# Attention and token/channel mixer on one core: w_ch1 fetched and split earlier, x split in the last two pairs, token products between the last turns

## The chip, the cores and the metric

The kernel runs on one core of one Trainium2 chip. The metric is device time in microseconds (us), the median of the timed executions. Engines are called PE (matmul), ACT, DVE, POOL (GpSimd) and SP (here only a DMA queue).

## The reference

Attention comes first, for 4 batches of 8 heads with 576 rows of 64 columns, all float32:

```python
q_rot, k_rot = (rotate(q), rotate(k))
scores = scale * np.matmul(q_rot, k_rot.transpose(0, 1, 3, 2))
scores = scores - np.max(scores, axis=-1, keepdims=True)
attn = np.exp(scores)
attn = attn / (np.sum(attn, axis=-1, keepdims=True) + 1e-09)
x = np.matmul(attn, v)            # heads side by side: 4 x 576 x 512
```

Then a mixer, with w_tok1 576x256, w_tok2 256x576, w_ch1 512x1536, w_ch2 1536x512:

```python
xt = x.transpose(0, 2, 1)
h = np.maximum(xt @ w_tok1, 0.0) @ w_tok2
u = x + h.transpose(0, 2, 1)
h2 = np.maximum(u @ w_ch1, 0.0) @ w_ch2
return u + h2
```

## The kernel before

**Two stages.** `attention` works through 16 pairs of heads (p = 0 to 15). `mixer` then works through 4 batches. Each engine has its own instruction list, written out by hand; there is no planner. Engines meet only at semaphores.

**One pair.** A pair has nine score tiles, i = 0 to 8. For each, PE makes the scores (`score`, L589 and L593), DVE takes the row maximum (`maximum`, L801), ACT the exponent (`exponent`, L715), PE turns the result (`turn`, ten transposes, L531), ACT and DVE copy the two halves out of PSUM (`copy_up` L724, `copy_low` L810), and PE multiplies by v (`values`, twenty matmuls, L633). There is one pair of banks for turned tiles: `turn` of a tile waits until both copies of the tile before are done. Tiles 7 and 8 are turned within the next pair's scores. The turned q of pair p+1 passes through `copy_q` (ACT, L705) and a DMA `moved_q` issued by SP (`move`, L422), and the first score of pair p+1 waits for that DMA. SP also waits in its list for `copy_v` (POOL, L500), to load v of pair p+1, ahead of these moves.

**Exact products out of rounded parts.** A float32 product of the mixer is made of three passes: operands are split into a rounded part ("hi", an ACT copy to float32r, `split_hi`) and the rest ("lo", a subtraction, `split_lo`, on DVE or POOL). `ChannelWeights` holds w_ch1: eight half chunks come by DMA (L156), `split_hi` (L162) rounds each half, `split_lo` (L169) subtracts a whole chunk of 128x1536. `TokenProducts` holds batch 0's x: five tiles t = 0 to 4, `split_hi` L204, `split_lo` L209 (L213 for the last, half one), and `products` (L221 to L224, six matmuls of 512 columns a tile, four for the last).

**The handover.** After the pair loop PE does: turn 7, values 5 and 6, products of x tiles 0 and 1, turn 8, values 7 and 8, products of x tiles 2 to 4. Then the mixer: `h_hi` (ACT, L1307) and `h_lo` (DVE, `token_lo`, L1494) read these sums; `u_unit` 0 to 3 (five transposes L1141, then twelve matmuls L1148); `hidden(0)` (L1116 to L1118), whose chunk c waits for `u_lo` of chunk c (DVE, L1500) and for `split_lo` of w_ch1's chunk c. SP loads w_ch2 in the meantime and POOL forms sums of it (L1091).

**Where the w_ch1 work lies.** The loads are issued in pairs 4 to 11. ACT rounds chunks 0 and 1 in pairs 13 and 14, chunks 2 and 3 after the loop. POOL subtracts chunks 0 and 1 at the end of pairs 14 and 15. DVE subtracts chunk 2 at the end of attention and chunk 3 within the mixer, between `u_lo` 1 and `u_lo` 2. The place of chunks 2 and 3 of w_ch1's rounded part is shared with `prob_a`, the exponents of tiles 0 to 4.

**Where the x work lies.** ACT rounds tiles 0 and 1 in pair 15 (tile 0 after `copy_up` of tile 8, tile 1 at its end, ahead of `copy_up` 6), the others after the loop. POOL subtracts tiles 0 and 1, DVE tiles 2 to 4.

Of the kernel before, what the change touches and what calls it, by code (L numbers as in the profile page):

```python
# [17 lines left out]
P = 128  # L18
# [43 lines left out]
def build(nc, q, k, v, w_tok1, w_tok2, w_ch1, w_ch2, rope, x_scratch, out):  # L62
    with ExitStack() as whole:
# [13 lines left out]
        w_ch1_lo = sb(whole, "w_ch1_lo", [P, CT, CH], F32R)  # L77
        with ExitStack() as placed:
            sb(placed, "w_ch1_first", [P, CT // 2, CH])
            prob_a = sb(placed, "prob_a", [P, CT // 2 * CH])  # L80
        wc1 = [sb(whole, "w_ch1_hi", [P, CT, CH], F32R), w_ch1_lo]
# [27 lines left out]
        with ExitStack() as ctx:  # L109
            first = attention(nc, ctx, whole, sb, slot, rest, ident, stage_or_x, raw_qk, rope_sb, rope_half, prob_a, token, wt1,  # L110
                              wt2, w1, x_stored, q, k, v, w_tok1, w_tok2, w_ch1, rope, x_scratch)
# [29 lines left out]

Attention = namedtuple("Attention", "sync gpsimd tensor scalar vector last_store buffers_left values_left slot_left")
Mixer = namedtuple("Mixer", "sync gpsimd tensor scalar vector first_token_hi")
# [83 lines left out]

def attention(nc, ctx, whole, sb, slot, rest, ident, stage_or_x, raw_qk, rope_sb, rope_half, prob_a, token, wt1, wt2, w1, x_stored,
              q, k, v, w_tok1, w_tok2, w_ch1, rope, x_scratch):
# [25 lines left out]
    MOVED_COLS = {"q": (slice(0, W), slice(0, W)), "k": (slice(HALF, S), slice(0, HALF))}  # L255
    sb(ctx, "spare_too", [P, 4576])

# [143 lines left out]
    def sync(sp):  # L401
# [45 lines left out]
        for p in range(N):  # L447
            if not no(p + 1):
                sp.wait_ge(v_copied, 2 * p + 2)
                load("v", p + 1)  # L450
            if not no(p + 1):
                sp.wait_ge(scores, p * TILES + G + 1)
            move("k", 0, p + 1)
            move("q", 0, p + 1)
            store(p - 1)
            load_next("k", p + 3)
            sp.wait_ge(scores, (p + 1) * TILES)
            move("k", 1, p + 1)
            move("q", 1, p + 1)
            load_next("q", p + 3)  # L460
            if 1 <= p <= len(chunks):
                for dst, part in chunks[p - 1][0]:
                    sp.dma_start(dst, part).then_inc(w_in[p - 1], 16)
            if 4 <= p < 4 + 2 * CT:
                w1.load(sp, w_ch1, (p - 4) // 2, p % 2)
            if p == 10:

                sp.wait_ge(x_stored, STORED * HP)
                sp.wait_ge(w_lo_done, len(PIECES))
                token.load_x(sp, 0, range(0, 2), ())  # L470
            if p == 11:
                token.load_x(sp, 0, range(2, HP), ())
            if p == 12:
                token.load_x(sp, 0, ())

    def gpsimd(pool):
# [35 lines left out]
        for p in range(N):  # L512
            copy_v(p, "B")
            if not no(p + 2):
                rotate(pool, "k", p + 2)
            copy_v(p + 1, "A")
            if not no(p + 2):
                rotate(pool, "q", p + 2)
            if p == N - 1:
                token.split_lo(pool, 0, 0)  # L520
                token.split_lo(pool, 0, 1)
            if 3 <= p < 3 + len(PIECES):
                weights_lo(p - 3)
            if N - 2 <= p < N:
                w1.split_lo(pool, p - (N - 2))

    def tensor(pe):
# [143 lines left out]

        first, p = slot[0], N
        turn(p - 1, 7)
        values(p - 1, 5)
        values(p - 1, 6)
        pe.wait_ge(exped, N * TILES - 1)
        token.products(pe, 0, 0, first).then_inc(token.x_used, 1)
        token.products(pe, 0, 1, first).then_inc(token.x_used, 1)
        turn(p - 1, 8)
        values(p - 1, 7)  # L680
        values(p - 1, 8)
        token.products(pe, 0, 2, first).then_inc(token.x_used, 1)
        token.products(pe, 0, 3, first).then_inc(token.x_used, 1)
        token.products(pe, 0, 4, first).then_inc(token.sums_ready, 1)

    def slot_left(pe, k):
# [9 lines left out]
    def scalar(act, h1_of_batch_0):  # L696
# [43 lines left out]
        for p in range(N):  # L740
            exponent(p, 0)
            exponent(p, 1)
            copy_up(p - 1, 8)
            if N - 3 <= p < N - 1:
                w1.split_hi(act, p - (N - 3), 0)
            if p == N - 1:
                act.wait_ge(products, 4 * N)
                token.split_hi(act, 0, 0)
            exponent(p, 2)
            copy_up(p, 0)  # L750
            exponent(p, 3)
            copy_up(p, 1)
            copy_up(p, 2)
            exponent(p, 4)
            copy_up(p, 3)
            exponent(p, 5)
            exponent(p, 6)
            copy_q(p + 1)
            copy_up(p, 4)
            exponent(p, 7)  # L760
            copy_up(p, 5)
            exponent(p, 8)
            if 3 <= p < 3 + len(PIECES):
                weights_hi(p - 3)
            if N - 3 <= p < N - 1:
                w1.split_hi(act, p - (N - 3), 1)
            if p == N - 1:
                token.split_hi(act, 0, 1)
            copy_up(p, 6)
            copy_up(p, 7)  # L770

        p = N
        token.split_hi(act, 0, 2)
        copy_up(p - 1, 8)
        token.split_hi(act, 0, 3)
        token.split_hi(act, 0, 4)
        w1.split_hi(act, 2, 0)
        w1.split_hi(act, 2, 1)
        w1.split_hi(act, 3, 0)
        act.wait_ge(token.sums_ready, 1)  # L780
        h1_of_batch_0(act)
        w1.split_hi(act, 3, 1)

    def vector(dve):
# [26 lines left out]

        def guard(p, h):
            if no(p):
                return
            t0, t1 = HEADS[h]
            dve.wait_ge(o_added, p * TILES + t1)
            dve.tensor_tensor(guarded[p % 2][:, t0:t1], output(h)[:, :, D], eps[:, t0:t1], ALU.add).then_inc(guard_done, 1)

        def invert(p, h):
            if no(p):  # L820
                return
            t0, t1 = HEADS[h]
            dve.wait_ge(guard_done, 2 * p + "AB".index(h) + 1)
            dve.reciprocal(inverse[p % 2][:, t0:t1], guarded[p % 2][:, t0:t1]).then_inc(inv_done, 1)

        def normalise(p, h):
            if no(p):
                return
            a, (t0, t1) = "AB".index(h), HEADS[h]
            dve.wait_ge(inv_done, 2 * p + a + 1)  # L830
            if p > 0:
                dve.wait_ge(x_stored, p * STORED)
            dve.tensor_tensor(x_pair[:, 1 - a:NG, a, :], output(h)[:, :, 0:D],
                              inverse[p % 2][:, t0:t1].unsqueeze(2).broadcast_to([P, t1 - t0, D]), ALU.mult).then_inc(x_done, 1)

        dve.memset(raw["q"][0:TAIL, 1, G, :], 0.0).then_inc(zero_halves, 1)
# [11 lines left out]
        for p in range(N):  # L848
            maximum(p, 0)
            copy_low(p - 1, 7)  # L850
            maximum(p, 1)
            normalise(p - 1, "A")
            copy_low(p - 1, 8)
            maximum(p, 2)
            maximum(p, 3)
            copy_low(p, 0)
            guard(p - 1, "B")
            copy_low(p, 1)
# [5 lines left out]
            copy_low(p, 3)  # L864
            invert(p - 1, "B")
            normalise(p - 1, "B")
            copy_low(p, 4)
            maximum(p, 7)
            maximum(p, 8)
            copy_low(p, 5)  # L870
            guard(p, "A")
            copy_low(p, 6)
            invert(p, "A")

        p = N
        copy_low(p - 1, 7)
        normalise(p - 1, "A")
        copy_low(p - 1, 8)
        token.split_lo(dve, 0, 2)
        token.split_lo(dve, 0, 3)  # L880
        guard(p - 1, "B")
        invert(p - 1, "B")
        token.split_lo(dve, 0, 4)
        normalise(p - 1, "B")
        w1.split_lo(dve, 2)

# [9 lines left out]
    def buffers_left(sp):  # L896

        sp.wait_ge(scores, N * TILES)

    def values_left(pool):  # L900

        pool.wait_ge(o_added, N * TILES)

    return Attention(sync=sync, gpsimd=gpsimd, tensor=tensor, scalar=scalar, vector=vector,
                     last_store=last_store, buffers_left=buffers_left, values_left=values_left, slot_left=slot_left)


def mixer(nc, ctx, sb, slot, ident, h, h1, pieces, token, wt2, wc1, w1, w1_sums, w1_parts, h_early, x_stored, first, w_ch1, w_ch2,
# [580 lines left out]
    def vector(dve):  # L1489
# [126 lines left out]

        token_lo(0, slot[0])

        def body(b, begins=False, last=False):
            if begins:  # L1620
                for c in range(CT):
                    u_lo(b, c)
                    if c == 1:
                        w1.split_lo(dve, 3)
                for n in range(len(WEIGHTS)):
                    w2_lo(n)
                los(b, 0, 3)
                add_u(b, 0)
            else:
                shares(b)  # L1630
# [132 lines left out]
```

## Time and profile before

| what | us |
|---|---|
| median of 3 runs | 621.48 (621.3 to 623.23) |
| profiled execution, its own time | 619.15 |
| its span (first to last instruction) | 617.2 |
| PE busy | 595.7 (97%) |
| DVE busy | 443.9 (72%) |
| ACT busy | 387.3 (63%) |
| POOL busy | 274.6 (44%) |

The profiled execution was 2.33 us shorter than the median, and 1.95 us of it lie outside the span. The granted clock was 0.998 of full speed. Attention ends and the mixer begins at about 275 us of the span. PE's busy time includes matmuls that overlap, so 97% tells only that its gaps are few.

### The profile page before, as it was taken

The page shows a single profiled execution, that of the slowest core. Times are in us where ns is not written, and L with a number is a line of the kernel's source. Part 1 is how long each engine was busy: PE and PEld are TensorE (multiplying, and loading weights), DVE is VectorE, ACT ScalarE, POOL GpSimd, SP SyncE. Part 2 cuts the span into 40 slices and gives each one's busy share as a digit, 9 for nine tenths or more (in the row PEclk, how much of TensorE's full clock was granted, in tenths as well). Part 3 has the DMA queues.
Part 4 walks back from the last instruction along what each step waited for, and adds up shares of the span by engine and source line. Part 5 has one row for each costly group of instructions (what it writes and reads, how often), then busy time and mean ns, then how long its engine had stood idle before and what let it go on. Part 6 is the DMA issues. An engine that isn't in the chain of part 4 may idle for free.

```text
span 617.2 us, 19511 instructions
## 1 busy us (share of the span) xinstructions
PE 595.7 (97%) x7796; PEld 543.1 (88%) x7796; DVE 443.9 (72%) x844; ACT 387.3 (63%) x725; POOL 274.6 (44%) x240
## 2 busy tenths in 40 slices
PE   2999999999999999989999999999999999999997
PEld 1788788788888888879999999999999999999996
DVE  5588788778888888855568876389735699364895
ACT  2566677776666677753736556775567766567753
POOL 4666677776666663348000016820038600168100
PEclk9999999999999999999999999999999999999999
DMA  4235445455456642270005320000310003200002
GB/s 136 74 95 152 127 110 135 133 136 137 135 137 171 169 127 72 58 235 1 1 1 205 86 77 1 1 2 6 107 51 0 0 0 85 78 0 1 1 2 78
DMA packets 49870, 48.18 MB, mean 78 GB/s; under 512 B 12800, under 2 KB 42048, under 8 KB 49792
## 3 DMA queue, kind: packets, MB, share of 16 engines
q1 hardware_dynamic: 49488, 47.00, 26.8%
q8 instruction: 58, 0.95, 0.6%
q14 instruction: 20, 0.16, 0.1%
q10 hardware_dynamic: 304, 0.07, 0.1%
HBM read 30.24 MB, written 9.44 MB: 64 GB/s over the span
## 4 chain that ended last, share of the span: by engine, by line
PE 93%; DVE 2%; DMA 1%; ACT 1%; issue 0%; DVEq 0%
PE rest L633 15%; PE slot L593 12%; PE rest L531 9%; PE slot L1116 8%; PE slot L1118 8%; PE slot L1117 8%; PE rest L1116 6%; PE rest L1118 6%; PE rest L1117 6%; PE slot L1148 2%; PE slot L531 2%; PE slot L589 2%; PE rest L1148 2%; DMA moved_q<-turned_q 1%; PE rest L224 1%; PE rest L221 1%
## 5 line engine op out<-in xcount | busy, mean ns | idle before, releaser
L801 DVE TENSOR_REDUCE neg_max<-slot 128x1 f32<-128x576 f32 x144 | 106.4, 755 | 21.6 <-PE slot L593 16.8
L1107 POOL TENSOR_TENSOR w_ch_part<-w_ch_sums,w_ch_part 128x512 fp32r<-128x512 f32 x21 | 31.0, 1476 | 180.3 <-ACT w_ch_part L1358 180.3
L1422 ACT ACTIVATE pieces<-h 128x288 fp32r<-128x288 f32 x168 | 73.8, 444 | 49.8 <-PE slot L1118 24.5
L633 PE MATMUL rest<-v,pt 128*64 128x65 f32 x2880 | 102.4, 225 | 0.0
L633 PEld LDWEIGHTS rest<-v,pt 128*64 128x64 f32 x2880 | 91.2, 138 | 10.6 <-ACT pt L724 6.2
L810 DVE COPY pt<-rest 128x320 f32<-128x320 f32 x144 | 70.1, 487 | 33.7 <-PE rest L531 33.2
L724 ACT ACTIVATE pt<-rest 128x320 f32<-128x320 f32 x144 | 62.7, 435 | 49.2 <-PE rest L531 48.2
L593 PE MATMUL slot<-turned_k,turned_q 64*128 64x288 f32 x256 | 86.3, 442 | 4.4 <-DMA moved_q<-turned_q 2.0
L593 PE MATMUL slot<-moved_k,moved_q 64*128 64x288 f32 x256 | 86.6, 443 | 0.0
L1513 DVE TENSOR_TENSOR pieces<-h,pieces 128x288 fp32r<-128x288 f32 x168 | 74.4, 453 | 9.3 <-ACT pieces L1422 8.8
L715 ACT ACTIVATE prob_a<-slot,neg_max 128x576 f32<-128x576 f32 x80 | 59.3, 741 | 17.5 <-DVE neg_max L801 14.4
L715 ACT ACTIVATE prob_b<-slot,neg_max 128x576 f32<-128x576 f32 x64 | 47.5, 742 | 12.9 <-DVE neg_max L801 10.3
L593 PEld LDWEIGHTS slot<-turned_k,turned_q 64*128 64x128 f32 x256 | 41.1, 192 | 10.0 <-ACT prob_a L715 4.4
L500 POOL COPY v<-raw_v 128x320 f32<-128x320 f32 x32 | 14.5, 452 | 78.4 <-PE rest L633 78.4
L531 PEld LDWEIGHTS rest<-ident,prob_a 64*128 64x128 f32 x800 | 35.0, 142 | 14.6 <-ACT pt L724 7.5
L593 PEld LDWEIGHTS slot<-moved_k,moved_q 64*128 64x128 f32 x256 | 41.1, 192 | 7.2 <-ACT turned_q L705 6.0
L1580 DVE TENSOR_TENSOR h<-h 128x288 f32<-128x288 f32 x96 | 42.6, 452 | 3.9 <-ACT h L1321 3.8
L361 POOL TENSOR_TENSOR by_sin<-raw_qk,rope_sb 128x640 f32<-128x640 f32 x29 | 44.9, 1550 | 0.0
L360 POOL TENSOR_TENSOR by_cos<-raw_qk,rope_sb 128x640 f32<-128x640 f32 x29 | 44.8, 1544 | 0.0
L531 PE MATMUL rest<-ident,prob_a 64*128 64x64 f32 x800 | 40.5, 230 | 0.8 <-ACT pt L724 0.8
L1358 ACT ACTIVATE w_ch_part<-w_ch_sums 128x512 fp32r<-128x512 f32 x42 | 26.5, 630 | 13.9 <-PE slot L1118 11.6
L531 PEld LDWEIGHTS rest<-ident,prob_b 64*128 64x128 f32 x640 | 28.1, 139 | 7.8 <-ACT pt L724 1.8
(236 smaller groups left out, 1761.3 us busy)
## 6 DMA issues: line engine op xcount, KB each, us to landing
moved_q<-turned_q SPq DMA_DIRECT2D x31, 160.0 KB, 2.7
raw_qk<-in_q_dram SPq DMA_DIRECT2D x16, 256.0 KB, 2.7
raw_v<-in_v_dram SPq DMA_DIRECT2D x16, 256.0 KB, 2.9
x_scratch<-x_pair SPq DMA_DIRECT2D x16, 256.0 KB, 2.7
stage_or_x<-x_scratch SPq DMA_DIRECT2D x16, 256.0 KB, 4.1
raw_qk<-in_k_dram SPq DMA_DIRECT2D x15, 256.0 KB, 2.9
w_ch_whole<-in_moe_w_ch_dram SPq DMA_DIRECT2D x8, 384.0 KB, 3.5
w_ch_A_whole<-in_moe_w_ch_dram SPq DMA_DIRECT2D x4, 768.0 KB, 7.8
```

The source lines that it names most:

```text
L531: return pe.matmul(to, x, ident[rows, rows], start=True, stop=True, is_transpose=True, skip_group_check=True)
L593: mm = pe.matmul(s[:, r, 0:HALF], x[:, cols], w, start=True, stop=True, skip_group_check=True)
L633: mm = pe.matmul(to[cols], pt_of(p, i)[:, j, cols], w, start=(j == 0), stop=(j == G), skip_group_check=True)
L715: act.activation(prob[i].rearrange("p (f n) -> p f n", f=2), score_slot(p, i)[:, :, 0:HALF], ACT.Exp, bias=neg_max[p % 2][:, i:i + 1]).the ...
L724: act.activation(pt_of(p, i)[:, :, top], rest[:, 0, 0:NG * D].rearrange("p (j n) -> p j n", j=NG), ACT.Copy).then_inc(up_done, 1)
L801: dve.tensor_reduce(neg_max[p % 2][:, i:i + 1], score_slot(p, i)[:, :, 0:HALF], AX.XY, ALU.max, negate=True).then_inc(maxed, 1)
L810: dve.tensor_copy(pt_of(p, i)[:, :, low], rest[:, 1, 0:NG * D].rearrange("p (j n) -> p j n", j=NG)).then_inc(low_done, 1)
L1116: pe.matmul(ps, lhs[0], rhs[0], start=first, stop=False, skip_group_check=True)
L1117: pe.matmul(ps, lhs[0], rhs[1], start=False, stop=False, skip_group_check=True)
L1118: return pe.matmul(ps, lhs[1], rhs[0], start=False, stop=last, skip_group_check=True)
L1422: act.activation(pieces[:, ring(m), 0, :], source[WEIGHTS[n]][:, ft, :], ACT.Copy).then_inc(piece_hi, 1)
L1513: dve.tensor_tensor(pieces[:, ring(m), 1, :], source[WEIGHTS[n]][:, ft, :], f32(pieces[:, ring(m), 0, :]), ALU.subtract).then_inc(piece_lo, 1)
```

## The change

1. `prob_a` gets a place of its own, so that w_ch1's chunks 2 and 3 can be rounded while attention runs. The load of w_ch2 waits also for turn 4 of the last pair.
2. The loads of w_ch1 are issued in pairs 3 to 10.
3. ACT rounds one chunk of w_ch1 in each of pairs 12 to 15: the first half after `copy_up` 8 of the pair before, the second at the end of the pair (in pair 15 behind `copy_up` 7).
4. POOL subtracts all four chunks, at the ends of pairs 13, 14 and 15 and after the loop. DVE subtracts none.
5. ACT rounds x tile 0 in pair 14 before exponent 5 and tile 1 at pair 14's end; tile 2 in pair 15 before exponent 5, tile 3 before `copy_up` 4, tile 4 after the loop. POOL subtracts tiles 0 to 3 (two in each of pairs 14 and 15), DVE tile 4. In pair 15 `copy_up` 6 is ahead of exponent 8.
6. PE, after the loop: products of tile 0, turn 7, values 5 and 6, products of tile 1, turn 8, products of tiles 2 to 4, values 7 and 8.
7. DVE's guard, reciprocal and normalisation of the last head run after the mixer's `token_lo`.

The diff, cut to its core:

```diff
-        with ExitStack() as placed:
-            sb(placed, "w_ch1_first", [P, CT // 2, CH])
-            prob_a = sb(placed, "prob_a", [P, CT // 2 * CH])
...
-    sb(ctx, "spare_too", [P, 4576])
+    sb(ctx, "spare_too", [P, 4576 - NG * S])
+    prob_a = sb(ctx, "prob_a", [P, NG * S])
...
-            if 4 <= p < 4 + 2 * CT:
-                w1.load(sp, w_ch1, (p - 4) // 2, p % 2)
+            if 3 <= p < 3 + 2 * CT:
+                w1.load(sp, w_ch1, *divmod(p - 3, 2))
...
-            if p == N - 1:
-                token.split_lo(pool, 0, 0)
-                token.split_lo(pool, 0, 1)
+            if p >= N - 2:
+                for t in range(2):
+                    token.split_lo(pool, 0, 2 * (p - (N - 2)) + t)
...
-            if N - 2 <= p < N:
-                w1.split_lo(pool, p - (N - 2))
+            if p > N - CT:
+                w1.split_lo(pool, p - (N - CT) - 1)
+        w1.split_lo(pool, CT - 1)
...
         first, p = slot[0], N
+        pe.wait_ge(exped, N * TILES - 1)
+        token.products(pe, 0, 0, first).then_inc(token.x_used, 1)
         turn(p - 1, 7)
         values(p - 1, 5)
         values(p - 1, 6)
-        pe.wait_ge(exped, N * TILES - 1)
-        token.products(pe, 0, 0, first).then_inc(token.x_used, 1)
         token.products(pe, 0, 1, first).then_inc(token.x_used, 1)
         turn(p - 1, 8)
-        values(p - 1, 7)
-        values(p - 1, 8)
         token.products(pe, 0, 2, first).then_inc(token.x_used, 1)
         token.products(pe, 0, 3, first).then_inc(token.x_used, 1)
         token.products(pe, 0, 4, first).then_inc(token.sums_ready, 1)
+        values(p - 1, 7)
+        values(p - 1, 8)
...
-            if N - 3 <= p < N - 1:
-                w1.split_hi(act, p - (N - 3), 0)
-            if p == N - 1:
-                act.wait_ge(products, 4 * N)
-                token.split_hi(act, 0, 0)
+            if p >= N - CT:
+                w1.split_hi(act, p - (N - CT), 0)
...
             copy_up(p, 3)
+            if p == N - 2:
+                act.wait_ge(products, 4 * N)
+                token.split_hi(act, 0, 0)
+            if p == N - 1:
+                token.split_hi(act, 0, 2)
             exponent(p, 5)
             exponent(p, 6)
             copy_q(p + 1)
+            if p == N - 1:
+                token.split_hi(act, 0, 3)
             copy_up(p, 4)
             exponent(p, 7)
             copy_up(p, 5)
+            if p == N - 1:
+                copy_up(p, 6)
             exponent(p, 8)
             if 3 <= p < 3 + len(PIECES):
                 weights_hi(p - 3)
-            if N - 3 <= p < N - 1:
-                w1.split_hi(act, p - (N - 3), 1)
+            if N - CT <= p < N - 1:
+                w1.split_hi(act, p - (N - CT), 1)
+            if p == N - 2:
+                token.split_hi(act, 0, 1)
+            if p < N - 1:
+                copy_up(p, 6)
+            copy_up(p, 7)
             if p == N - 1:
-                token.split_hi(act, 0, 1)
-            copy_up(p, 6)
-            copy_up(p, 7)
+                w1.split_hi(act, CT - 1, 1)
 
         p = N
-        token.split_hi(act, 0, 2)
+        token.split_hi(act, 0, 4)
         copy_up(p - 1, 8)
-        token.split_hi(act, 0, 3)
-        token.split_hi(act, 0, 4)
-        w1.split_hi(act, 2, 0)
-        w1.split_hi(act, 2, 1)
-        w1.split_hi(act, 3, 0)
         act.wait_ge(token.sums_ready, 1)
         h1_of_batch_0(act)
-        w1.split_hi(act, 3, 1)
...
         normalise(dve, p - 1, "A")
+        dve.wait_ge(token.x_lo_done, G)
+        token.split_lo(dve, 0, G)
         copy_low(p - 1, 8)
-        token.split_lo(dve, 0, 2)
-        token.split_lo(dve, 0, 3)
-        guard(p - 1, "B")
-        invert(p - 1, "B")
-        token.split_lo(dve, 0, 4)
-        normalise(p - 1, "B")
-        w1.split_lo(dve, 2)
+
+    def last_output(dve):
+        for step in (guard, invert, normalise):
+            step(dve, N - 1, "B")
...
         sp.wait_ge(scores, N * TILES)
+        sp.wait_ge(turned, (N - 1) * TILES + G + 1)
...
         token_lo(0, slot[0])
+        first.last_output(dve)
...
-                    if c == 1:
-                        w1.split_lo(dve, 3)
```

## Rows read from the trace of the kernel before

**Rows 1.** The page: the chain that ended last, by engine
```profile
PE 93%; DVE 2%; DMA 1%; ACT 1%; issue 0%; DVEq 0%
```

**Rows 2.** Waits of PE, whole span: who for whom, us in total, times, longest
```profile
PE slot L593 <- DMA moved_q<-turned_q: 2.0, 2, 1.3
PE rest L531 <- ACT pt L724: 1.6, 2, 0.9
...
PE slot L1116 <- DVE ut_lo L1500: 1.0, 1, 1.0
PE slot L1148 <- DVE h_lo L1494: 0.9, 1, 0.9
```

**Rows 3.** Timeline of PE, 246 to 296: start, us, engine, line, operation, tiles, [idle before]
```profile
263.63 0.53 PE L531 MATMUL rest<-ident,prob_b 64*128 64x64 f32 x10
265.02 0.53 PE L531 MATMUL rest<-ident,prob_b 64*128 64x64 f32 x10 [0.86 <-ACT pt L724]
265.47 1.39 PE L633 MATMUL rest<-v,pt 128*64 128x65 f32 x40
266.79 0.50 PE L221 MATMUL slot<-x_parts,w_tok_hi 128*128 128x512 f32 x1
267.13 0.40 PE L223 MATMUL slot<-x_parts,w_tok_hi 128*128 128x512 f32 x1
...
269.78 0.53 PE L531 MATMUL rest<-ident,prob_b 64*128 64x64 f32 x10
...
275.51 0.71 PE L1141 MATMUL slot<-ident,stage_or_x 128*128 128x128 f32 x5
277.09 0.39 PE L1148 MATMUL slot<-w_tok_hi,h_hi 128*128 128x256 f32 x1 [0.87 <-DVE h_lo L1494]
...
278.78 0.71 PE L1141 MATMUL slot<-ident,stage_or_x 128*128 128x128 f32 x5
279.24 0.36 PE L1148 MATMUL slot<-w_tok_hi,h_hi 128*128 128x256 f32 x1
...
286.51 0.30 PE L1117 MATMUL slot<-ut_lo,w_ch_hi 128*128 128x288 f32 x1
286.65 0.29 PE L1118 MATMUL slot<-ut_hi,w_ch_lo 128*128 128x288 f32 x1
287.92 0.40 PE L1116 MATMUL slot<-ut_hi,w_ch_hi 128*128 128x288 f32 x1 [0.98 <-DVE ut_lo L1500]
```

**Rows 4.** Timeline of DVE, 216 to 300
```profile
282.60 4.53 DVE L169 TENSOR_TENSOR w_ch_lo<-w_ch_whole,w_ch_hi 128x1536 fp32r<-128x1536 f32 x1
```

**Rows 5.** Timeline of POOL, 216 to 300
```profile
240.06 0.45 POOL L500 COPY v<-raw_v 128x320 f32<-128x320 f32 x1 [1.10 <-PE rest L633]
...
281.99 3.54 POOL L1091 TENSOR_TENSOR w_ch_S_whole<-w_ch_S_whole,w_ch_A_whole 128x1536 f32<-128x1536 f32 x1
```

**Rows 6.** Timeline of ACT, 216 to 300
```profile
245.86 0.70 ACT L705 ACTIVATE turned_q<-slot 128x640 f32<-128x640 f32 x1 [0.23 <-PE slot L531]
...
249.83 0.45 ACT L724 ACTIVATE pt<-rest 128x320 f32<-128x320 f32 x1
...
261.08 0.44 ACT L724 ACTIVATE pt<-rest 128x320 f32<-128x320 f32 x1 [0.29 <-PE rest L531]
...
264.00 0.64 ACT L204 ACTIVATE x_parts<-stage_or_x 128x512 fp32r<-128x512 f32 x1
264.52 0.45 ACT L724 ACTIVATE pt<-rest 128x320 f32<-128x320 f32 x1
```

**Rows 7.** Timeline of PE, 244 to 252: turn 7 of pair 14
```profile
250.41 0.50 PE L531 MATMUL rest<-ident,prob_b 64*128 64x64 f32 x10
```

**Rows 8.** POOL's subtractions of w_ch1 chunks: ns min/median/max, first and last start
```profile
L169 POOL TENSOR_TENSOR w_ch_lo<-w_ch_whole,w_ch_hi x2: 3458/3470/3482, 249.6 to 265.9; 128x1536 fp32r<-128x1536 f32 x2
```

**Rows 9.** The 62 moves of turned q and k (L422)
```profile
DMA to landing us min/median/max: 1.9/2.7/4.8
```

**Rows 10.** Timeline of SP's queue, 40 to 80
```profile
60.03 2.53 SPq L432 DMA_DIRECT2D x_scratch<-x_pair  x2
```

More of the change, by code:

```diff
@@ L109, in build @@
         with ExitStack() as ctx:
-            first = attention(nc, ctx, whole, sb, slot, rest, ident, stage_or_x, raw_qk, rope_sb, rope_half, prob_a, token, wt1,
+            first = attention(nc, ctx, whole, sb, slot, rest, ident, stage_or_x, raw_qk, rope_sb, rope_half, token, wt1,
                               wt2, w1, x_stored, q, k, v, w_tok1, w_tok2, w_ch1, rope, x_scratch)
@@ L139, in _ @@
                     then.vector(dve)
-Attention = namedtuple("Attention", "sync gpsimd tensor scalar vector last_store buffers_left values_left slot_left")
+Attention = namedtuple("Attention", "sync gpsimd tensor scalar vector last_output last_store buffers_left values_left slot_left")
 Mixer = namedtuple("Mixer", "sync gpsimd tensor scalar vector first_token_hi")
@@ L225, in products, with attention @@
         return mm
-def attention(nc, ctx, whole, sb, slot, rest, ident, stage_or_x, raw_qk, rope_sb, rope_half, prob_a, token, wt1, wt2, w1, x_stored,
+def attention(nc, ctx, whole, sb, slot, rest, ident, stage_or_x, raw_qk, rope_sb, rope_half, token, wt1, wt2, w1, x_stored,
               q, k, v, w_tok1, w_tok2, w_ch1, rope, x_scratch):
@@ L764, in scalar, with guard, invert, normalise @@
                 weights_hi(p - 3)
-            if N - 3 <= p < N - 1:
-                w1.split_hi(act, p - (N - 3), 1)
+            if N - CT <= p < N - 1:
[5 more added lines that the diff above has]
+            copy_up(p, 7)
             if p == N - 1:
-                token.split_hi(act, 0, 1)
-            copy_up(p, 6)
-            copy_up(p, 7)
+                w1.split_hi(act, CT - 1, 1)
         p = N
-        token.split_hi(act, 0, 2)
+        token.split_hi(act, 0, 4)
         copy_up(p - 1, 8)
-        token.split_hi(act, 0, 3)
-        token.split_hi(act, 0, 4)
-        w1.split_hi(act, 2, 0)
-        w1.split_hi(act, 2, 1)
-        w1.split_hi(act, 3, 0)
         act.wait_ge(token.sums_ready, 1)
         h1_of_batch_0(act)
-        w1.split_hi(act, 3, 1)
+    def guard(dve, p, h):
+        if no(p):
+            return
+        t0, t1 = HEADS[h]
+        dve.wait_ge(o_added, p * TILES + t1)
+        dve.tensor_tensor(guarded[p % 2][:, t0:t1], output(h)[:, :, D], eps[:, t0:t1], ALU.add).then_inc(guard_done, 1)
+    def invert(dve, p, h):
+        if no(p):
+            return
+        t0, t1 = HEADS[h]
+        dve.wait_ge(guard_done, 2 * p + "AB".index(h) + 1)
+        dve.reciprocal(inverse[p % 2][:, t0:t1], guarded[p % 2][:, t0:t1]).then_inc(inv_done, 1)
+    def normalise(dve, p, h):
+        if no(p):
+            return
+        a, (t0, t1) = "AB".index(h), HEADS[h]
+        dve.wait_ge(inv_done, 2 * p + a + 1)
+        if p > 0:
+            dve.wait_ge(x_stored, p * STORED)
+        dve.tensor_tensor(x_pair[:, 1 - a:NG, a, :], output(h)[:, :, 0:D],
+                          inverse[p % 2][:, t0:t1].unsqueeze(2).broadcast_to([P, t1 - t0, D]), ALU.mult).then_inc(x_done, 1)
     def vector(dve):
@@ L810, in copy_low @@
             dve.tensor_copy(pt_of(p, i)[:, :, low], rest[:, 1, 0:NG * D].rearrange("p (j n) -> p j n", j=NG)).then_inc(low_done, 1)
[L812 to L834, printed above, removed]
         dve.memset(raw["q"][0:TAIL, 1, G, :], 0.0).then_inc(zero_halves, 1)
@@ L851, in vector @@
             maximum(p, 1)
-            normalise(p - 1, "A")
+            normalise(dve, p - 1, "A")
             copy_low(p - 1, 8)
@@ L856, in vector @@
             copy_low(p, 0)
-            guard(p - 1, "B")
+            guard(dve, p - 1, "B")
             copy_low(p, 1)
@@ L864, in vector @@
             copy_low(p, 3)
-            invert(p - 1, "B")
-            normalise(p - 1, "B")
+            invert(dve, p - 1, "B")
+            normalise(dve, p - 1, "B")
             copy_low(p, 4)
@@ L870, in vector @@
             copy_low(p, 5)
-            guard(p, "A")
+            guard(dve, p, "A")
             copy_low(p, 6)
-            invert(p, "A")
+            invert(dve, p, "A")
         p = N
         copy_low(p - 1, 7)
-        normalise(p - 1, "A")
+        normalise(dve, p - 1, "A")
+        dve.wait_ge(token.x_lo_done, G)
+        token.split_lo(dve, 0, G)
         copy_low(p - 1, 8)
-        token.split_lo(dve, 0, 2)
-        token.split_lo(dve, 0, 3)
-        guard(p - 1, "B")
-        invert(p - 1, "B")
-        token.split_lo(dve, 0, 4)
-        normalise(p - 1, "B")
-        w1.split_lo(dve, 2)
+    def last_output(dve):
+        for step in (guard, invert, normalise):
+            step(dve, N - 1, "B")
     def last_store(sp):
@@ L904, in attention @@
     return Attention(sync=sync, gpsimd=gpsimd, tensor=tensor, scalar=scalar, vector=vector,
-                     last_store=last_store, buffers_left=buffers_left, values_left=values_left, slot_left=slot_left)
+                     last_output=last_output, last_store=last_store, buffers_left=buffers_left, values_left=values_left, slot_left=slot_left)
 def mixer(nc, ctx, sb, slot, ident, h, h1, pieces, token, wt2, wc1, w1, w1_sums, w1_parts, h_early, x_stored, first, w_ch1, w_ch2,
```

## Prediction

> **What bounds the kernel now.** I read the chain of waits first: 93% of it is PE [rows 1], so only PE's gaps and added PE work can move the time. The second view is PE's waits: beside start-up it waits 2.0 us for the `moved_q` DMA (two times), 1.6 for ACT's copies, 1.0 for `ut_lo` and 0.9 for `h_lo` [rows 2]. The third view is PE's timeline about 275 us, where three of these gaps stand in one handover: 0.86, 0.87 and 0.98 us [rows 3]. Everything that the change moves on ACT, DVE and POOL is off the chain, unless it closes one of these or opens a new one. So the sum has at most some 3 us to win out of 619.15 us of the profiled execution (span 617.2 and 1.95 around it). The median was 2.33 above that execution; I carry the difference over unchanged.
>
> **Gap one, before turn 7.** Turn 7 waits for `copy_up` 6, and ACT has exponent 8 and the rounding of x tile 1 ahead of it. Turn 6 starts at 263.63; a turn gives way to the next work after 0.45 (265.02 to 265.47), so PE is free at 264.08 and starts at 265.02 [rows 3]: 0.94 lost. Afterwards products of tile 0 stand there. They need exponent 7, which ACT has finished before 264.00 [rows 6], and x tile 0 split in pair 14. They last longer than the copy that turn 7 then waits for, which now goes ahead of exponent 8. Gain 0.94.
>
> **Gap two, before the first mixer products.** The sums are followed by the five transposes at 275.51. In the next unit the L1148 matmuls follow their transposes after 0.46 (278.78 to 279.24), here after 1.58 (275.51 to 277.09), because ACT's `h_hi` and DVE's `h_lo` come between [rows 3]: 1.12 lost. Afterwards values 7 and 8 follow the sums. They are 40 matmuls of the kind that took 1.32 (265.47 to 266.79), and with 0.46 of transposes this covers 1.78, more than the 1.58 needed [rows 3]. Gain 1.12. With ACT free of w_ch1 and DVE's last-head steps behind `token_lo`, nothing is queued before the two splits. What is late next is x_done for unit 3, about 1 us after `token_lo`, while PE needs it three units (over 6 us) on: hidden.
>
> **Gap three, in the first hidden tile.** Matmuls there follow each other after 0.14 (286.51, 286.65); the next comes at 287.92, so 1.13 is lost [rows 3]. It waits for `ut_lo` of chunk 2, which stands in DVE's list behind the subtraction of w_ch1's chunk 3, 282.60 to 287.13 [rows 4]. That subtraction goes to POOL, before the mixer. Chunk 2 is then ready long before, and chunk 3's splits have 2.4 us of hidden matmuls (18 by 0.13) to finish in. Gain 1.13. Sum of gains 0.94 + 1.12 + 1.13 = 3.19.
>
> **Cost one: one more switch of kind.** Products go in three blocks instead of two. The first product holds PE for 0.34 (266.79 to 267.13), the eleven behind it 0.24 each (267.13 to 269.78) [rows 3]: 0.10 to enter a block. Leaving one has no row of its own; from 0 to the 0.10 of entering, I take 0.1. Cost 0.2.
>
> **Cost two: x tile 1 at the end of pair 14.** The rounding of x tile 1 holds ACT for 0.52 (264.00 to 264.52), and PE's turn begins 0.05 after the copy behind it is over (264.52 + 0.45, against 265.02) [rows 3, 6]. In pair 14 the copy behind it is `copy_up` 6, now at 249.83 for 0.45 [rows 6]. Moved by 0.52 it ends at 250.80, and turn 7 can start at 250.85 instead of 250.41 [rows 7]. That is 0.44 on PE, the only engine without slack. The exponents of pair 15 behind it move along with PE and cost nothing more. The bounds are 0 (PE late for another reason) and the whole 0.52.
>
> **Other ACT insertions.** x tile 0 before exponent 5 of pair 14 uses 0.52, in front of exponents that wait for DVE's maxima anyway; ACT has another 0.23 idle before `copy_q` [rows 6]. I find `copy_q` unmoved. In pair 15, x tiles 2 and 3 move `copy_up` 4 (idle 0.29 before it [rows 6]) by about 0.3, to the very edge of turn 5. Value 0, at worst 0.3. w_ch1's first halves stand where such halves stand now in pairs 13 and 14, and the second halves of pairs 12 to 14 likewise, with no wait of PE among rows 2 that names them: 0. Pair 15's second half is behind `copy_up` 7 and covered by values and products.
>
> **POOL and SP.** The subtraction of chunk 0 (3.47 [rows 8]) now stands in pair 13 ahead of `copy_v` for pair 14, which ran at 240.06 [rows 5]; it comes out near 242.4. SP waits for it in order, then issues v's load and pair 15's `moved_k`, both now near 243 to 245, and only then `moved_q`, which waits for `copy_q` (ends 246.56 [rows 6]) anyway. So the queue isn't late, but v's load is now just ahead of `moved_q`. That DMA lands after 2.7 at the median and 4.8 at worst [rows 9], and at 2.7 it lands just as PE wants it. I take 0, since a stall here would hide the 0.44 of cost two; the upper end is 2.1 - 0.4 = 1.7. POOL's sums of w_ch2 start when their loads land and values 8 is over, about as before. The added wait for turn 4 on SP is over before the last score, for which SP waits already: 0. w_ch1's loads keep their number and size; one lands beside pair 4's start instead of one beside pair 12's: 0 to the 1.3 of the longest such stall [rows 2]. Moving `prob_a` changes no instruction.
>
> **A rule against the change.** DVE's subtraction of 4.53 ran while POOL's L1091 was busy to 285.53 (281.99 + 3.54), and ended 1.60 after that [rows 4, 5]: it had stood still until POOL was done. The Trainium skill, "SBUF — State Buffer", section "Who interferes with whom", has the rule: a DVE operation with two SBUF inputs and a GpSimd operation that reads SBUF exclude each other for a whole instruction, and which starts second waits. These rows agree. After the change only DVE's split of x tile 4 meets POOL (its last chunk): POOL from about 267.9 to 271.3, DVE then at most 1.60 more, to 272.9, and products of tile 4 come near 273.0. If instead the two ran side by side, the split would be there at about 270, with the same sum.
>
> **Sum.** 3.19 - 0.2 - 0.44 = 2.55 us. Profiled execution 616.6; median 621.48 - 2.55 = 618.9.
>
> **Rivals.**
> (a) Forecast: 618.9, its own range 618.1 to 619.8 (gaps counted only as PE's idle, 2.71, give 2.07).
> (b) Pair 14's `copy_up` isn't late for PE: no cost two, 618.5. For it: other second halves cost nothing. Against: 0.13 between copy and turn is all the slack there is [rows 6, 7].
> (c) `moved_q` of pair 15 takes the place of cost two: landing at 4.8 instead of 2.7, PE waits 2.1; 3.19 - 0.2 - 2.1 = 0.9, 620.6. For it: the same DMA stopped PE twice already [rows 2]. Against: v's load is nearly done by then.
> (d) The exclusion between DVE and POOL is worse than I place it: DVE blocked past 273.0 holds `copy_low` 8 and PE too, by up to 1.6, so 620.5. Against: it needs POOL's last subtraction some 0.7 later than its inputs allow. This is the mechanism of the Trainium skill's section above.
> (e) The change doesn't do what it says at gap one, as x tile 0 is not split in time or turn 7 is late anyway: 0.94 stays, 619.9.
> (f) Slower: the two PE stalls on `moved_q` go with slow stretches of SP's queue (two small stores took 2.53 [rows 10]). One DMA more from pair 3 on shifts which issue falls on such a stretch. At 1.3 a stall [rows 2] it decides from two further stalls on (2.6 against 2.55); four further ones make 5.2 - 2.55 = 2.65 more, 624.1. For it: every pair's start hangs on this DMA. Against: 13 of 15 starts passed without a stall.
>
> **How the numbers follow.** A measurement of this kernel can tell about 0.3% from no change, 1.9 us. Chances: (a) 0.49, (b) 0.12, (c) 0.18, (d) 0.05, (e) 0.08, (f) 0.08. Under 619.6 lie (b) and most of (a): faster 0.59. Between 619.6 and 623.3 lie the rest of (a), (c), (d), (e) and the milder (f): same 0.33. Slower 0.08. The range takes (b) with one of the two present stalls gone at the low end (618.5 - 1.3 = 617.2), and (c) with a stall more at the upper end (620.6 + 1.3): 617.2 to 621.9.
>
> **What would show it.** PE's timeline after 263 without the three idle marks; a mark of about 0.4 on turn 7 of pair 14, released by `pt` L724; `moved_q` marks no more than two; DVE's x tile 4 split at about 3 us where POOL's L169 runs. Wrong would be: a PE wait on `h_lo` or `ut_lo` left over, idle time on pair starts above 2 us, or PE gaps in the rest of the mixer grown by what the handover gave.

## The result, and the profile after

| | before | after |
|---|---|---|
| median, us | 621.26 (618.29 to 623.23, 17 runs) | 616.55 (614.72 to 620.05, 17 runs) |
| ratio | | 0.9932, 95% interval 0.9915 to 0.9948 |
| profiled execution: its own time, span | 619.15, 617.2 | 618.23, 616.1 |

The kernel became faster, by more than forecast: 616.55 lies below the range of 617.2 to 621.9. The medians differ by 4.71 us, the means by 4.29. The two profiled executions differ by only 1.1 us in span, so neither the size of the gain nor its cause can be read from two spans. They have to be read stage by stage.

Waits of PE in the kernel after, whole span (who for whom, us in total, times, longest):

```profile
PE slot L592 <- DMA moved_q<-turned_q: 2.9, 3, 1.4
...
PE rest L530 <- ACT pt L723: 1.0, 2, 0.8
```

Against [rows 2], the waits on `h_lo` and `ut_lo` are gone and `pt` fell from 1.6 to 1.0. But `moved_q` rose from 2.0 to 2.9 in this execution: a third pair start was hit. That hides part of the gain from whoever compares spans only. It also goes against two signs that the prediction set for itself: no more than two such marks, and no more than 2 us idle at pair starts.

The same handover as in [rows 3, 7], in PE's timeline of the kernel after (start, us, engine, line, operation, tiles, [idle before]):

```profile
251.27 0.48 PE L592 MATMUL slot<-turned_k,turned_q 64*128 64x288 f32 x1
252.77 0.52 PE L530 MATMUL rest<-ident,prob_b 64*128 64x64 f32 x10 [0.26 <-ACT pt L723]
...
266.01 0.53 PE L530 MATMUL rest<-ident,prob_b 64*128 64x64 f32 x10
266.47 0.50 PE L218 MATMUL slot<-x_parts,w_tok_hi 128*128 128x512 f32 x1
268.05 0.53 PE L530 MATMUL rest<-ident,prob_b 64*128 64x64 f32 x10
...
269.82 0.50 PE L218 MATMUL slot<-x_parts,w_tok_hi 128*128 128x512 f32 x1
...
271.42 0.53 PE L530 MATMUL rest<-ident,prob_b 64*128 64x64 f32 x10
271.87 0.49 PE L218 MATMUL slot<-pieces,w_tok_hi 128*128 128x512 f32 x1
...
275.74 1.39 PE L632 MATMUL rest<-v,pt 128*64 128x65 f32 x40
277.05 0.77 PE L1145 MATMUL slot<-ident,stage_or_x 128*128 128x128 f32 x5
277.57 0.36 PE L1152 MATMUL slot<-w_tok_hi,h_hi 128*128 128x256 f32 x1
```

The marks of 0.86, 0.87 and 0.98 have no successor here, and one new mark of 0.26 stands on turn 7 of pair 14.

**One measure for the handover.** To keep pair starts out of the comparison I take the stretch from ACT's `copy_q` of pair 15 to ACT's first `hidden_out`. Before, `copy_q` starts at 245.86 [rows 6]; the other end of the stretch in ACT's timeline before, and then both ends after:

```profile
289.81 0.66 ACT L1321 ACTIVATE h<-slot 128x576 f32<-128x576 f32 x1 [3.70 <-PE slot L1118]
```

```profile
247.78 0.70 ACT L704 ACTIVATE turned_q<-slot 128x640 f32<-128x640 f32 x1
289.03 0.66 ACT L1325 ACTIVATE h<-slot 128x576 f32<-128x576 f32 x1 [2.44 <-PE slot L1122]
```

That is 43.95 before and 41.25 after: 2.70 us gained, against a forecast of 2.55. From there to the end of the span it is 327.39 and 327.07. Everything ahead of it cost 1.92 more in this execution: 0.88 before the first `copy_q` of the span (27.35 before, 28.23 after; 0.51 of it at the very start), and 1.04 between that and the `copy_q` of pair 15, most of it (0.95) in the pair whose start waited at 204.98.

DVE and POOL in the kernel after, at the end of attention:

```profile
270.41 3.51 DVE L210 TENSOR_TENSOR x_parts<-stage_or_x,x_parts 64x512 fp32r<-64x512 f32 x1 [0.97 <-ACT x_parts L201]
273.96 0.49 DVE L837 COPY pt<-rest 128x320 f32<-128x320 f32 x1
```

```profile
244.20 0.47 POOL L498 COPY v<-raw_v 128x320 f32<-128x320 f32 x1
...
269.87 3.50 POOL L166 TENSOR_TENSOR w_ch_lo<-w_ch_whole,w_ch_hi 128x1536 fp32r<-128x1536 f32 x1 [1.24 <-ACT w_ch_hi L159]
```

DVE's split of x tile 4 starts 0.54 after POOL's last chunk and ends 0.55 after it (273.92 against 273.37). The prediction had placed this meeting.

### The profile page after: what moved, and what is told of

The parts are those of the page before. It is cut to its first block, busy times and chain, and to the rows that moved or that the text cites. A ratio compares the mean times of both kernels' runs of the same rounds, so it can differ in the third digit from the quotient of the medians.

```text
span 616.1 us, 19512 instructions
## 1 busy us (share of the span) xinstructions
PE 595.9 (97%) x7796; PEld 543.1 (88%) x7796; DVE 439.6 (71%) x840; ACT 386.6 (63%) x725; POOL 282.0 (46%) x244
## 4 chain that ended last, share of the span: by engine, by line
PE 94%; DMA 2%; ACT 1%; DVE 1%; issue 0%; DVEq 0%
PE rest L632 15%; PE slot L592 11%; PE rest L530 8%; PE slot L1120 8%; PE slot L1122 8%; PE slot L1121 8%; PE rest L1120 6%; PE rest L1122 6%; PE rest L1121 6%; PE slot L1152 2%; PE rest L1152 2%; PE slot L530 2%; DMA moved_q<-turned_q 2%; PE slot L588 2%; PE rest L221 1%; PE rest L218 1%
```

## The experiments

"Stretch" is the measure above, from each kernel's own ACT timeline. Ratios are to before, timed on the same chip in the same series of runs.

**e1, the changed kernel again.** 

> The changed kernel once more. Theory H (the handover alone): the handover gives 2.7 us, and the rest of the measured 4.2 us is the chance of which executions were timed; ratio to before 0.9955. Theory S (a systematic second gain): ratio 0.993 again, and fewer or shorter PE waits on moved_q at pair starts than before has. In this trace as in the first: a wait of about 0.3 us on turn 7 of pair 14 released by pt, DVE's x tile 4 subtraction at about 3.5 us, no waits of PE on h_lo or ut_lo.

Measured: 617.24 against 620.42, ratio 0.9955 (0.9932 to 0.9978), stretch 41.24, the wait on turn 7 0.25. The ratio is theory H's number, and PE's waits on `moved_q` were not fewer or shorter than before's, as theory S wanted (three, 2.6 us, against two, 2.0). But the interval still overlaps the first one (0.9915 to 0.9948), so this alone doesn't settle it.

**e2, prob_a's place alone.** The edit:

```diff
-            prob_a = sb(placed, "prob_a", [P, CT // 2 * CH])
...
+    prob_a = sb(ctx, "prob_a", [P, NG * S])
...
+        sp.wait_ge(turned, (N - 1) * TILES + G + 1)
```

> The kernel before with prob_a at its new place and SP's added wait for turn 4 of the last pair, nothing else. Theory H: ratio 1.000, within 0.1%. Theory S by the place of prob_a: ratio 0.997.

Measured: ratio 1.0018 (0.9995 to 1.0041), stretch 43.94 with the three old marks (0.86, 0.87, 0.96). The place gives nothing (at most 0.05% by the interval); it only permits the rest.

**e3, the loads alone.** The edit:

```diff
-            if 4 <= p < 4 + 2 * CT:
-                w1.load(sp, w_ch1, (p - 4) // 2, p % 2)
+            if 3 <= p < 3 + 2 * CT:
+                w1.load(sp, w_ch1, *divmod(p - 3, 2))
```

> The kernel before with the w_ch1 loads issued in pairs 3 to 10 instead of 4 to 11, nothing else. Theory H: ratio 1.000. Theory S by the loads: ratio 0.997, with about 1.5 us less PE wait on moved_q in the median execution. Rival from the prediction (slow stretches of SP's queue shift by one DMA, to the worse): over 1.000, with a wait at a third pair start.

Measured: ratio 1.0002 (0.9974 to 1.0029), the three old marks again (0.86, 0.86, 1.00). The stretch is 44.91 here, because it holds a wait of 0.89 on `moved_q` at pair 15's start; without the 0.97 that this adds it is before's. The profiled execution had PE waits on `moved_q` at four pair starts, 3.0 us in sum, and still the median didn't move. Neither the gain by the loads nor my rival (f) is there beyond 0.3%.

**e4, the loads late in the changed kernel.** As the changed kernel, with the load of pair 3 issued in pair 4 beside pair 4's own. 

> The changed kernel with the w_ch1 loads in pairs 4 to 10, two of them in pair 4. Theory H: as the changed kernel, ratio 0.9955. Theory S by the loads: 1.5 us slower than the changed kernel of this call.

Measured: 617.15, ratio 0.9959 (0.9932 to 0.9986), stretch 41.23. As e1 (0.9955): the place of the loads is worth nothing beyond 0.3%.

**e5, PE's order back.** The edit, after the pair loop:

```diff
-        pe.wait_ge(exped, N * TILES - 1)
-        token.products(pe, 0, 0, first).then_inc(token.x_used, 1)
         turn(p - 1, 7)
...
+        pe.wait_ge(exped, N * TILES - 1)
+        token.products(pe, 0, 0, first).then_inc(token.x_used, 1)
         token.products(pe, 0, 1, first).then_inc(token.x_used, 1)
         turn(p - 1, 8)
+        values(p - 1, 7)
+        values(p - 1, 8)
...
-        values(p - 1, 7)
-        values(p - 1, 8)
```

> The changed kernel with PE's own order of before after the loop: turn 7, values 5 and 6, products 0 and 1, turn 8, values 7 and 8, products 2 to 4. Read from the trace as the stretch from copy_q of pair 15 to the first hidden_out: 43.95 us before, 41.25 with the change. Theory (the three gaps): gap one returns in part, 0.6 (copy_up 6 is no longer behind exponent 8), gap two whole, 1.1, less 0.2 for the third block of products: 42.75. Rival (ACT's and DVE's relief closed the gaps, PE's order is worth nothing): 41.25 to 41.5.

Measured: ratio 0.9978 (0.9955 to 1.0), stretch 43.52 (247.76 to 291.28). PE's marks after the loop:

```profile
267.15 0.53 PE L530 MATMUL rest<-ident,prob_b 64*128 64x64 f32 x10 [0.64 <-ACT pt L723]
273.69 0.81 PE L632 MATMUL rest<-v,pt 128*64 128x65 f32 x20 [0.51 <-DVE pt L837]
279.80 0.39 PE L1152 MATMUL slot<-w_tok_hi,h_hi 128*128 128x256 f32 x1 [0.87 <-DVE h_lo L1498]
```

Gaps one and two return as expected (0.64, 0.87). The third mark wasn't expected: DVE's `copy_low` 8 stands behind the split of x tile 4, which here starts at 271.37, takes 1.65 and meets the end of POOL's chunk, while `values` 8 no longer has products ahead of it. Start to start gap one costs 0.71 here, gap two 1.11 and the third mark 0.66, less the 0.2 to 0.3 of the third block of products. So 2.3 us of the 2.7 hang on PE's order, more than the 1.5 I gave it, and part of that is cover for a DVE delay that the change itself makes.

**e6, chunk 3 back on DVE.** The edit:

```diff
-        w1.split_lo(pool, CT - 1)
...
                     u_lo(b, c)
+                    if c == 1:
+                        dve.wait_ge(w1.lo_done, CT - 1)
+                        w1.split_lo(dve, CT - 1)
```

> The changed kernel with w_ch1's chunk 3 subtracted by DVE between u_lo 1 and u_lo 2, as before, and not by POOL. Theory as predicted (gap three goes with this instruction): the stretch grows by 1.1, a PE wait on ut_lo returns. Rival (it was POOL's busy instruction at that moment that made 1.6 us into 4.53, by the exclusion): DVE's subtraction now meets the end of POOL's second sum instead of the start of its third, takes about 2.8, chunk 2 is ready 0.5 before PE wants it, and the stretch stays at 41.25.

Measured: ratio 0.9966 (0.9947 to 0.9985), stretch 41.25, no mark on `ut_lo`. The rival is right, to its 2.8 us. DVE, then POOL, in this kernel:

```profile
281.91 2.75 DVE L166 TENSOR_TENSOR w_ch_lo<-w_ch_whole,w_ch_hi 128x1536 fp32r<-128x1536 f32 x1
284.58 1.69 DVE L1503 TENSOR_TENSOR ut_lo<-rest,ut_hi 128x256 fp32r<-128x256 f32 x4
```

```profile
276.08 6.96 POOL L1094 TENSOR_TENSOR w_ch_S_whole<-w_ch_A_whole 128x1536 f32<-128x1536 f32 x2 [8.63 <-PE rest L631]
283.00 5.04 POOL L1094 TENSOR_TENSOR w_ch_S_whole<-w_ch_S_whole,w_ch_A_whole 128x1536 f32<-128x1536 f32 x1
```

The same instruction that took 4.53 in [rows 4] takes 2.75 here: it waits about 1.1 for POOL's second sum to end at 283.04, works, and POOL's third sum stands still in its turn (5.04 against 3.54 in [rows 5]). With DVE free at 284.66, PE has both `ut_lo` in time. So gap three wasn't the price of this instruction on DVE, but of its start 0.6 us behind the start of a POOL sum (282.60 against 281.99 before).

**e7, x tile 1 moved and a later wait for moved_q.** As e9 below, and

```diff
-            elif i == 0:
-                pe.wait_ge(tiles_in[0], p * MOVED)
...
                 for r, (x, w) in enumerate(...):
+                    if i == 0 and p > 0 and r == 1:
+                        pe.wait_ge(tiles_in[0], p * MOVED)
```

> The changed kernel with x tile 1 rounded in pair 15 between copy_up 1 and copy_up 2 (POOL subtracts it in pair 15), and with the wait for moved_q in score 0 moved behind the matmul that doesn't need it. Theory: cost two (0.25 us on turn 7 of pair 14) is gone, the stretch is 41.0; each PE wait on moved_q shrinks by up to 0.4. Ratio to before 0.994. Rival: the wait inside the tile parts two matmuls that ran side by side, and each pair gets 0.2 longer: ratio 0.999.

Measured: 617.97, ratio 0.9964 (0.9951 to 0.9978), stretch 41.93, which contains a wait of 0.52 on `moved_q` at pair 15's start. PE's marked waits on `moved_q` were 1.1 us in sum, and undisturbed pairs took 15.3 to 15.4 us, no longer than the 15.3 to 15.5 of the changed kernel. So undisturbed pairs don't show the rival's loss. Pairs that wait do lose more than their marks say: the stretch is 1.16 longer than e9's (40.77) with a mark of 0.52, and from one `copy_q` to the next it takes 16.16 over pair 3's start, against 15.39 undisturbed, with no mark at all. The fall of the marks is therefore no proof that the waits shrank, and the time shows no gain either: 0.9964 beside e1's 0.9955. Inconclusive.

**e8, values 5 ahead of score 0.** As e9, and

```diff
+            values(p - 1, 5)
             score(p, 0)
             score(p, 1)
             turn(p - 1, 7)
-            values(p - 1, 5)
             values(p - 1, 6)
```

> As the one before without the moved wait, but values 5 of the pair before stands ahead of score 0, so that moved_q has 0.66 us more to land. Theory: PE's waits on moved_q (2 to 3 us in an execution) nearly go: ratio 0.992. Rival: the copies between turn 7 and turn 8 and the exponents for score 2 have too little cover, 0.1 to 0.3 lost in each of 15 pairs: ratio 0.996 to 1.000.

Measured: 624.97, ratio 1.0078 (1.0057 to 1.0099): slower than either kernel. The waits on `moved_q` did shrink, to 1.1 in sum. But every pair takes 16.16, as two `copy_q` in a row show:

```profile
222.12 0.70 ACT L704 ACTIVATE turned_q<-slot 128x640 f32<-128x640 f32 x1 [0.23 <-PE slot L530]
238.28 0.70 ACT L704 ACTIVATE turned_q<-slot 128x640 f32<-128x640 f32 x1 [0.23 <-PE slot L530]
```

The changed kernel has 15.43 there (216.90 to 232.33). The rival's direction, at more than twice its size: about 0.7 for each pair. 0.56 of it lies between turn 8 and turn 0, where scores 2 and 3 stand: 1.95 (244.75 to 246.70) against 1.39 in e9 (238.48 to 239.87). PE's timeline marks no idle time for it, since the profile's matmul ends overlap the next starts; only starts show it, and which wait it is stays open.

**e9, x tile 1 away from the end of pair 14.** The edit:

```diff
             copy_up(p, 1)
+            if p == N - 1:
+                token.split_hi(act, 0, 1)
             copy_up(p, 2)
...
-            if p == N - 2:
-                token.split_hi(act, 0, 1)
```

POOL's list goes along: it subtracts tile 0 in pair 14, and tiles 1, 2 and 3 in pair 15.

> The changed kernel with x tile 1 rounded in pair 15 between copy_up 1 and copy_up 2, and nothing else (POOL subtracts it in pair 15). Theory of cost two: the 0.25 us wait of PE on turn 7 of pair 14 is gone and no other comes, the stretch from copy_q of pair 15 to the first hidden_out is 41.0 instead of 41.25. Rival: another stall takes its place (copy_up 2 or POOL's later work) and it stays 41.25. In the time neither can be told from the changed kernel.

Measured: 616.39, ratio 0.9948 (0.9923 to 0.9973), stretch 40.77:

```profile
247.61 0.70 ACT L704 ACTIVATE turned_q<-slot 128x640 f32<-128x640 f32 x1
288.38 0.66 ACT L1325 ACTIVATE h<-slot 128x576 f32<-128x576 f32 x1 [2.44 <-PE slot L1122]
```

The mark is gone and the stretch is 0.47 shorter (41.24 to 40.77), not 0.25: the idle mark understates the stall, which start to start is about the 0.44 that the prediction gave it. In time it can't be told from the changed kernel, but it has the shortest handover of all.

**e10, the changed kernel a third time.** 

> The changed kernel a third time, to settle its distance from before. Theory H (2.7 us from the handover, the rest chance): 2.7 to 3 us, ratio 0.995 to 0.996. Theory S (a second systematic gain of 1.5 us that one comparison of 12 runs missed): ratio 0.993. The stretch is 41.25 again, and PE's waits on moved_q at pair starts are anything from 0 to 4 us in sum.

Measured: 616.77 against 620.16, ratio 0.9944 (0.9923 to 0.9965), stretch 41.24, PE's waits on `moved_q` 3.4 us in sum. The ratio lies between the two theories and its interval holds both; it decides nothing by itself and counts in the sum over all series below.

**e11, copy_up 6 behind exponent 8 again.** The edit:

```diff
-            if p == N - 1:
-                copy_up(p, 6)
             exponent(p, 8)
+            if p == N - 1:
+                copy_up(p, 6)
```

> The changed kernel with copy_up 6 of pair 15 behind exponent 8, as it was before. Theory (products of tile 0, 1.6 us, cover both orders): copy_up 6 moves from 266.6 to about 266.8 and ends long before the 1.6 us of products; the stretch stays 41.25. Rival (ACT's order closed gap one): a wait of PE on pt ahead of turn 7 returns, 41.5 or more.

Measured: 617.57, ratio 0.996 (0.9941 to 0.9978), stretch 41.24, no mark on turn 7. `copy_up` 6's place in ACT's list is worth nothing once products of tile 0 stand ahead of turn 7.

**The distance from before, over all series.** The changed kernel (three times), e4, e6 and e11 share the stretch of 41.2; e2 and, without its stall at pair 15, e3 share before's. Means of the one kind against the other within each series: 4.29 us less (17 against 17 runs), 2.81 (24 against 59, e2 and e3 counted with before), 2.35 (9 against 28), 3.03 (17 against 19). Weighted by their sizes that is 3.1, with a resampled 95% interval of 2.7 to 3.5. The three later series alone give 2.8. The first lies 1.5 above them, more than the spread within the series makes likely (standard errors about 0.5 and 0.2), and no run tells what made it so.

The handover gives 2.70 of the distance. About 0.3 more lies after the first `hidden_out`: 327.02 to 327.13 in the ten kernels from after on that hold the change (e7 and e8 included), 327.25 to 327.41 in before, e2 and e3. It is not in the mixer. From the first `hidden_out` to SP's last issue it is 323.70 to 323.79 in all thirteen profiles. That issue, before and after:

```profile
613.56 0.39 SPq L1085 DMA_DIRECT2D out_dram<-h  x1
```

```profile
612.73 0.39 SPq L1089 DMA_DIRECT2D out_dram<-h  x1
```

From there to the end of the span it is 3.64 before and 3.37 after (3.55 to 3.66 in before, e2 and e3, 3.29 to 3.37 in the ten others). Why the end comes sooner after the last store is open; e2 and e3 show that neither `prob_a`'s place nor the loads do it alone.

## Why the prediction was right and where it failed

**Sum.** Right: 2.55 forecast, 2.70 on the stretch. Start to start its terms are 0.94 + 1.06 + 1.25 - 0.27 - 0.45, and 0.17 that the sum didn't have.

**Gap one.** Right: 0.94 forecast, no mark left; e5 brings 0.64 back, and e11 shows that products of tile 0 alone cover it.

**Gap two.** Right: transposes to first product are 0.52 after (277.05 to 277.57), against 1.58 before: 1.06 for the forecast 1.12.

**Gap three.** The size was nearly right: the next matmul waits no longer, and the first hidden tile takes 3.36 from its first matmul to `hidden_out` (285.67 to 289.03) against 4.61 (285.20 to 289.81), so 1.25 for the forecast 1.13. The reason was only half right. I wrote that it "goes to POOL" and so the gap goes. e6 leaves the subtraction on DVE and has no gap either. What made it was DVE starting just behind a POOL sum; with the other changes DVE reaches this instruction 1.44 us earlier after `copy_q` (36.74 before, 35.30 in e6), and that shifts the meeting.

**Cost one.** Forecast 0.2. Three blocks take 1.58, 1.60 and 3.87, 7.05 together, against 2.99 and 3.79 in two blocks before (266.79 to 269.78, 271.72 to 275.51): 0.27. The last `values` gave 0.17 back (1.31 instead of 1.48).

**Cost two.** Right: 0.44 forecast, 0.45 measured. Score 0 of pair 15 to turn 7 takes 1.50 (251.27 to 252.77), against 1.05 before (249.36 to 250.41), and e9 gets 0.47 back.

**Other ACT insertions, POOL and SP.** Right at 0. From turn 7 of pair 14 to turn 6 of pair 15 it is 13.24 (252.77 to 266.01), against 13.22 before (250.41 to 263.63). `copy_v` moved to 244.20 and `moved_q` of pair 15 followed `copy_q` as before, with no wait at that pair's start in any of the seven profiles that have this order (after, e1, e4, e5, e6, e10, e11).

**The rule on DVE and POOL.** This case's traces agree with the Trainium skill, "SBUF — State Buffer", section "Who interferes with whom", by which the later of two such instructions on DVE and GpSimd waits for the other's end: 3.51 for a DVE subtraction that takes 0.69 in e6, where POOL is idle, and 1.65 where it meets only the end. It was covered, by 0.8 us (273.92 against products of tile 4 at 274.74), and e5 shows the price of 0.51 when the cover is gone. My rival (d) named this mechanism, `copy_low` 8 included; it didn't decide because the cover held.

**What failed: the step from the profiled execution to the median, and the range.** I put the median 2.33 above the profiled execution, by three runs (621.48), carried that over unchanged, and let the range end at 617.2, with one stall fewer. Both were too narrow. `moved_q` stalls change from execution to execution of one kernel: 2.9, 2.6 and 3.4 us in three profiles of the changed kernel, and 0.9 in e2 against 2.0 in before, which has the same attention loop. Single runs of before spread from 615.92 to 624.29, and its median over longer series was 620.16 to 621.26, 0.2 to 1.3 below my base. The changed kernel's later medians were 617.24 (just inside the range) and 616.77 (again below it); before's 620.42 and 620.16 of those series, less 2.7 and 0.3, are 617.4 and 617.2.

Of the 2.4 us between 618.9 and 616.55, 0.15 is the handover, 0.3 the end of the span, which was not in the sum at all, and 0.2 the base as this series measured it. The other 1.7 is what the first comparison shows beyond the later ones. It may be an upward draw, but nothing here shows its cause: with the right base the sum would have met the later series and not the first.

Two smaller slips. The signs at pair starts (no more than two marks, no more than 2 us) were set from one profile. They were passed although the handover did what was forecast: 2.4 to 4.1 us in after, e1, e4, e5, e6, e9, e10 and e11, against 2.0, 0.9 and 3.0 in before, e2 and e3. These are too few to tell whether the change adds to the stalls; the times leave little room for it, with 3.1 gained against 2.7 + 0.3. And the chances give 0.08 to slower, which is all of rival (f), while the same sentence counts its milder part under "same".

## What to carry to other kernels

When a handover between stages has several short idle marks, look for ready work of the busy engine to put in front of each waiting instruction; taking PE's new order back cost 2.3 of 2.7 us here. The order alone, put into the kernel before, wasn't run, so how much of the rest of the change it needs is open; POOL had x tile 0 split there by 257.2 (255.89 + 1.27), well ahead of turn 7. Compare such changes by a stretch between two landmarks, since the span mixes in waits that change from run to run. Before moving a DVE subtraction elsewhere because it looks slow, see which POOL instruction it overlaps: a shift of one microsecond can do as much.

## What the runs showed of the hardware

One DVE subtraction (128x1536, both inputs in SBUF) took 4.53 or 2.75 us, depending on when POOL's started. POOL's took 5.04 instead of 3.54 when DVE was ahead of it. A smaller one took 0.69, 1.65 or 3.51.

Pair starts that waited on `moved_q` sit at nearly the same spots of the span in all profiles, about 47 us or three pairs apart: at 61.8 to 64.5 in all but e7 (which loses time there without a mark), then in some of them near 110, 156, 204 and 250, with a few smaller ones between. In 28 of the 29 marked waits over 0.5 us SP's queue is slow there. In the kernel after, around 204:

```profile
201.38 0.49 SPq L420 DMA_DIRECT2D moved_q<-turned_q  x1
201.91 0.58 SPq L427 DMA_DIRECT2D x_scratch<-x_pair  x1
202.54 2.00 SPq L430 DMA_DIRECT2D x_scratch<-x_pair  x2
```

```profile
204.98 0.48 PE L592 MATMUL slot<-turned_k,turned_q 64*128 64x288 f32 x1 [0.73 <-DMA moved_q<-turned_q]
```

The two small stores take 2.00 where 1.10 to 1.13 is usual, as in [rows 10]; over all profiles the slow ones take 1.88 to 2.88. The exception is e9 at 109.94, where they took 1.10. Whether something recurs in time or with every third pair is open: in e8, whose pairs are longer, the two marks are 48.8 apart. Beside the start-up this is PE's largest wait left.
